# Attention's beginning in an attention, routed-experts and feed-forward kernel: the first head's operands written by engines, loads on two queues, hash operand in four operations, some thresholds behind the statistics

## The chip, the cores and the metric

The kernel runs on one core of one Trainium2 chip. The metric is the time of one execution on the device in microseconds (us), taken as the median of several runs. The chip has a tensor engine (PE), a vector engine (DVE), a scalar engine (ACT), GpSimd (POOL) and a sync engine (SP) whose queue only issues transfers here. Results of matrix products land in PSUM, everything else is kept in SBUF.

## The reference

Three stages follow one another; the change is in the first.

```python
def _attn_ref(q, k, v, proj):              # q, k, v: (2, 8, 768, 64), proj: (64, 6)
    q_bits = (einsum('bhsd,dk->bhsk', q, proj) > 0)
    k_bits = (einsum('bhsd,dk->bhsk', k, proj) > 0)
    mask = q_bucket[:, :, :, None] == k_bucket[:, :, None, :]     # bucket: the six bits as a number
    scores = where(mask, q @ k.T / sqrt(64), -1e9)
    attn = exp(scores - max); attn = attn / (sum(attn) + 1e-09)
    return attn @ v
...
x = attention output as (1536, 512)
x = moe(x)      # top 2 of 8 experts, 512 -> 1024 -> 512, gate with noise
return ffn(x)   # 512 -> 2048 -> 512, g = h * sigmoid(1.702 h)
```

## The kernel before

Attention walks over 16 heads, taken as 8 pairs. A head is worked in 6 steps of 128 query rows, 96 steps in all; n counts them. Each step does `scores(n)` (4 products into PSUM, L721), `statistics(n)` on DVE (a row maximum, L1080, and the small exp_arg, L1083), an exponential on ACT (L1386), `transposes(n)` on PE (6 of 128x128, L732), and their copy out by ACT (L1395). In the loop over n, PE issues scores(n + 2), then transposes(n), then a unit of the next pair if one is due, then every second step the product with V for the head before (L746). ACT runs one exponential ahead of the copies.

Scores are made from four stacks per head, QA, KA, QB and KB, each 128 rows by 768 columns inside the big weight tile W. QA and KA hold the high and low parts of Q and K (each fp32 number is split in two), so that two products give nearly full precision; QB and KB hold in their upper 64 rows the hash bits, as 0 or a large number, which push rows of different buckets apart.

A pair's operands are made in 8 units. Units 0 and 1 transpose the two halves of Q (L703), 2 and 3 those of K; ACT copies the high part out of PSUM (L1380) and DVE the rest, `lo = ps - hi` (L1064). Units 4 to 7 multiply the parts with the hash operand `hash_m` (L708), and DVE compares the result with a threshold, once for each head of the pair, and writes it into QB or KB (L1074). The high and low parts are then moved into the stacks by 12 transfers of 192 KB per pair on SP's queue (L461); a pair's first scores wait for all of them. Pair 0's units run before the loop; those of pair p + 1 run in steps 0 to 7 of pair p (`unit_at`).

SP's queue issues in program order: Q and K of pair 0 (L411), the projection twice (L446, L447), router weights and noise (L448 to L450), then for each pair the 12 moves, the next pair's Q and K, V (L416) and one chunk of expert weights into `staged` (L422). GpSimd scales Q in place, once per pair (L533), and behind the scaling of pairs 0 to 3 splits one staged chunk into high and low parts (`split_chunk`, L522 and L527). Pair p's units therefore wait on PE for GpSimd's scaling, and this stands in GpSimd's order behind the split of the chunk before.

Semaphores named below: `s_ud` counts units done by DVE, `s_unit` units issued by PE, `s_hi` high parts done by ACT, `s_stq` and `s_stk` the moves landed.

## Time and profile before

| | |
|---|---|
| median of 3 runs | 957.33 us (955.73 to 957.73) |
| the profiled execution | 957.01 us, its span 955.1 us |
| busy in the span | PE 892.1 us (93%), DVE 393.9, ACT 412.0, GpSimd 320.4 |
| attention | from the start to about 303 us |

The span is what the trace covers; about 2 us of the execution lie around it. A busy PE is the union of its pipelined products, not PE at its peak. Times in rows are microseconds from the span's start. "PEclk" is the granted clock of TensorE as a share of full speed.

### The profile page before, as it was taken

The page shows a single profiled execution, that of the slowest core. Times are in us where ns is not written, and L with a number is a line of the kernel's source. Part 1 is how long each engine was busy: PE and PEld are TensorE (multiplying, and loading weights), DVE is VectorE, ACT ScalarE, POOL GpSimd, SP SyncE. Part 2 cuts the span into 40 slices and gives each one's busy share as a digit, 9 for nine tenths or more (in the row PEclk, how much of TensorE's full clock was granted, in tenths as well). Part 3 has the DMA queues.
Part 4 walks back from the last instruction along what each step waited for, and adds up shares of the span by engine and source line. Part 5 has one row for each costly group of instructions (what it writes and reads, how often), then busy time and mean ns, then how long its engine had stood idle before and what let it go on. Part 6 is the DMA issues. An engine that isn't in the chain of part 4 may idle for free.

```text
span 955.1 us, 13447 instructions
## 1 busy us (share of the span) xinstructions
PE 892.1 (93%) x4966; PEld 778.9 (82%) x4966; DVE 393.9 (41%) x758; ACT 412.0 (43%) x695; POOL 320.4 (34%) x214
## 2 busy tenths in 40 slices
PE   2699999999999889999999999998899999999998
PEld 2566666676665689999999999998789998989986
DVE  4477676767774732122221222212233333333322
ACT  1576676676675323343443434421443323223222
POOL 1222020000060035676646566479564110100100
PEclk8699999999999979999999999999799999999999
DMA  7346525623432014666565544444343010000000
GB/s 157 98 124 171 122 79 142 169 69 84 116 111 86 26 41 142 200 200 222 173 198 190 179 160 155 138 155 130 119 157 89 33 44 22 33 0 0 34 1 33
DMA packets 69747, 105.13 MB, mean 110 GB/s; under 512 B 33364, under 2 KB 35412, under 8 KB 69684
## 3 DMA queue, kind: packets, MB, share of 16 engines
q1 hardware_dynamic: 56240, 74.32, 27.0%
q0 software_dynamic: 5488, 15.51, 5.1%
q10 hardware_dynamic: 7956, 14.49, 4.5%
q8 instruction: 36, 0.59, 0.2%
q14 instruction: 27, 0.22, 0.1%
HBM read 64.61 MB, written 20.81 MB: 89 GB/s over the span
## 4 chain that ended last, share of the span: by engine, by line
PE 84%; DVE 6%; issue 3%; ACT 2%; SPq 2%; DMA 1%; POOL 1%; ACTq 0%; DVEq 0%; POOLq 0%
PE psS L864 15%; PE psS L1003 14%; PE psS L1018 9%; PE psS L882 7%; PE psV L746 7%; PE psT L732 5%; PE psS L721 5%; PE psV L1018 5%; PE psV L882 4%; PE psM L882 4%; DVE W L1074 2%; PE psM L708 2%; PE psT L897 1%; ACT probT L1395 1%; PE psM L703 1%
## 5 line engine op out<-in xcount | busy, mean ns | idle before, releaser
L527 POOL TENSOR_TENSOR W<-staged,W 128x1024 fp32r<-128x1024 f32 x80 | 191.4, 2394 | 133.1 <-ACT W L1455 115.3
L864 PE MATMUL psS<-xT_hi,W 128*128 128x416 f32 x512 | 142.2, 359 | 1.1 <-DVE xT_lo L1270 1.1
L1003 PE MATMUL psS<-x2T_hi,W 128*128 (+1 forms) x512 | 134.5, 344 | 3.9 <-issue 3.9
L1386 ACT ACTIVATE prob<-psS,exp_arg 128x768 f32<-128x768 f32 x96 | 95.5, 994 | 37.1 <-DVE exp_arg L1083 37.0
L1080 DVE TENSOR_REDUCE neg_max<-psS 128x1 f32<-128x768 f32 x96 | 91.5, 953 | 45.9 <-PE psS L721 45.0
L721 PE MATMUL psS<-W 128*128 128x384 f32 x384 | 94.4, 369 | 11.7 <-DMA W<-k_hi 10.0
L1395 ACT ACTIVATE probT<-psT 128x768 f32<-128x768 f32 x96 | 78.0, 812 | 59.0 <-PE psT L732 57.4
L1003 PEld LDWEIGHTS psS<-x2T_hi,W 128*128 128x128 f32 x512 | 94.7, 191 | 9.4 <-issue 4.2
L1276 DVE SCALAR_TENSOR_TENSOR hT_lo<-psS,hT_hi 128x416 fp32r<-128x416 f32 x64 | 37.9, 592 | 155.9 <-ACT hT_hi L1448 155.9
L721 PEld LDWEIGHTS psS<-W 128*128 128x128 f32 x384 | 65.5, 196 | 38.9 <-issue 34.8
L864 PEld LDWEIGHTS psS<-xT_hi,W 128*128 128x128 f32 x512 | 92.8, 188 | 2.3 <-issue 1.2
L1344 DVE TENSOR_TENSOR g_sb<-psS,sig 128x384 f32<-128x384 f32 x64 | 35.7, 558 | 140.5 <-ACT sig L1529 140.5
L864 PE MATMUL psS<-xT_lo,W 128*128 128x416 f32 x256 | 90.2, 352 | 0.0
L1529 ACT ACTIVATE sig<-psS 128x384 f32<-128x384 f32 x64 | 31.4, 491 | 134.4 <-PE psS L1003 134.4
L1003 PE MATMUL psS<-x2T_lo,W 128*128 (+1 forms) x256 | 87.4, 341 | 0.0
L732 PE MATMUL psT<-ident,prob 128*128 128x128 f32 x576 | 80.7, 277 | 5.6 <-ACT probT L1395 5.6
L1455 ACT ACTIVATE W<-staged 128x1024 fp32r<-128x1024 f32 x67 | 70.7, 1055 | 34.0 <-issue 20.5
L732 PEld LDWEIGHTS psT<-ident,prob 128*128 128x128 f32 x576 | 67.4, 142 | 16.4 <-issue 13.2
L1018 PE MATMUL psS<-W,g_hi 128*128 128x512 f32 x256 | 79.9, 393 | 0.3 <-issue 0.3
L522 POOL TENSOR_TENSOR W<-staged,ones_col 128x1024 fp32r<-128x1024 f32 x13 | 24.6, 1894 | 137.4 <-DMA staged<-in_moe_w 97.4
L882 PE MATMUL psS<-hT_hi,W 128*128 128x416 f32 x256 | 69.5, 353 | 0.0
L746 PE MATMUL psV<-probT,v_raw 128*64 128x384 f32 x360 | 68.0, 499 | 0.0
(258 smaller groups left out, 1410.1 us busy)
## 6 DMA issues: line engine op xcount, KB each, us to landing
staged<-in_moe_w SPq DMA_DIRECT2D x64, 512.0 KB, 3.6
ys_dram<-x_sb ACTq DMA_DIRECT2D x68, 208.0 KB
W<-q_hi SPq DMA_DIRECT2D x32, 192.0 KB, 3.3
W<-k_hi SPq DMA_DIRECT2D x32, 192.0 KB, 3.7
staged<-in_moe_w_in SPq DMA_DIRECT2D x8, 512.0 KB, 3.4
staged<-in_moe_w_out SPq DMA_DIRECT2D x8, 512.0 KB, 3.6
q_raw<-in_q SPq DMA_DIRECT2D x16, 192.0 KB, 4.0
k_raw<-in_k SPq DMA_DIRECT2D x16, 192.0 KB, 3.7
```

The costliest lines, as they stand in the source:

```text
L527: nc.gpsimd.tensor_tensor(W[:, at + BLOCK:at + BLOCK + CH], staged[:, n % 2], W[:, at:at + CH].bitcast(F32), ALU.subtract).then_inc(s_spli ...
L721: last = nc.tensor.matmul(psS[:, n % 2, half, 0:HALF], stack(slot, a)[:, qt * P:(qt + 1) * P], stack(slot, b_)[:, half * HALF:(half + 1) * ...
L732: last = nc.tensor.transpose(psT[:, half, j * P:(j + 1) * P], prob[:, n % 2, c * P:(c + 1) * P], ident[:])
L746: last = nc.tensor.matmul(av_bank(hd)[half * D:(half + 1) * D, 0:HALF], v_raw[:, hd // 2 % 2, hd % 2, c * D:(c + 1) * D], probT[:, hd % 2, ...
L864: mm = nc.tensor.matmul(psS[:, 0, f % 2, 0:TM], W[:, at:at + P], x[:, t % 2, c], start=c == 0 and n == 0, stop=c == DC - 1 and n == 2)
L882: mm = nc.tensor.matmul(y_bank[d][:, 0:TM], W[:, at:at + P], h[:, f % 2], start=f == 0 and n == 0, stop=f == FC - 1 and n == 2)
L1003: mm = nc.tensor.matmul(psS[:, 0, f % 2, 0:GN], W[:, at:at + P], x[:, bass.ds(buf + c * GN, GN)], start=c == 0 and n == 0, stop=c == DC - ...
L1018: mm = nc.tensor.matmul(out_bank[j], gp[:, f % 2, j * P:(j + 1) * P], W[:, at:at + DM], start=f == 0 and n == 0, stop=f == GC - 1 and n == 2)
L1080: nc.vector.tensor_reduce(neg_max[:, o, 0:1], psS[:, o, :, 0:HALF], mybir.AxisListType.XY, ALU.max, negate=True).then_inc(s_stat, 1)
L1386: nc.scalar.activation(prob[:, o, :].rearrange("p (a c) -> p a c", a=2), psS[:, o, :, 0:HALF], ACT.Exp, bias=exp_arg[:, o, 0:1], scale=exp ...
L1395: nc.scalar.activation(probT[:, hd % 2, :, t * P:(t + 1) * P].rearrange("p (a c) q -> p a c q", a=2), psT[:, :, 0:HALF].rearrange("p a (c ...
L1455: A(W[:, at:at + CH], staged[:, n % 2], ACT.Copy).then_inc(s_whi if block < E else s_late, 1)
```

## The change

Only the beginning of attention is rewritten, and the scaling of Q for all pairs.

- Scaling: GpSimd's in-place scaling of q_raw is gone. ACT's copy of the Q units takes `scale=SCALE`, and DVE's low part of Q becomes `ps * SCALE - hi` in one operation. PE's unit 0 waits for the Q transfers themselves.
- First loads: SP issues head 0's Q, half of the projection and head 0's K; ACT's queue issues head 1's Q, the other half and head 1's K. Pair 1's Q and K come next on SP's queue; V, router weights, noise and the first staged chunk come behind pair 0's moves.
- Hash operand: four DVE operations of 64 x 24 (with a `sign` tile set ahead) in place of sixteen of 64 x 6.
- Pair 0's units use a PSUM bank each. Head 0's stacks are written by engines: GpSimd copies Q's high part into both halves of QA, ACT K's parts into KA and KB, DVE Q's low part into QB. Head 1's six parts still go by transfer, and `moved(pr)` counts them; `scores(6)`, head 1's first, waits for them.
- Thresholds: those of head 0 come first, in 4 operations; those of head 1 are put behind the statistics of steps 0 and 1.
- Pair 1's units are one step later in the loop (steps 1 to 8). PE also does 6 products that nobody reads (`unread`) at its start and 3 ahead of `scores(0)`.

```diff
 def unit_bank(u, first):
-    return psS[:, u // 2 % 2, u % 2] if first else psM
+    return (psS[:, 0, 0], psS[:, 0, 1], psS[:, 1, 0], psS[:, 1, 1], psT[:, 0], psT[:, 1], psV, psM)[u] if first else psM
+
+def moved(pr):
+
+    return max(96 * pr - 48, 0)
 def columns(t, buf, j):
...
 def unit_at(n):
-    return n // PS + 1, n % PS
+    return n // PS + 1, n % PS - (n < PS)
 def attention_over(eng):
...
-    load_qk(0)
+    sp.dma_start(q_raw[:, :, 0], q_v[0].rearrange("p (t d) -> p t d", d=D)).then_inc(s_q, 16)
     sp.dma_start(proj_sb[0:D, :], proj).then_inc(s_proj, 16)
-    sp.dma_start(proj_sb[D:P, :], proj).then_inc(s_proj, 16)
-    sp.dma_start(w_router[:, :, 0:E], w_gate.rearrange("(c p) e -> p c e", p=P)).then_inc(s_wr, 16)
-    sp.dma_start(w_router[:, :, E:2 * E], w_noise.rearrange("(c p) e -> p c e", p=P)).then_inc(s_wr, 16)
-    sp.dma_start(noise_sb[:].rearrange("p (b t) e -> p b (t e)", b=B),
-                 noise.rearrange("(b p t) e -> p b (t e)", b=B, t=NT)).then_inc(s_wr, 16)
+    sp.dma_start(k_raw[:, :, 0], k_v[0].rearrange("p (t d) -> p t d", d=D)).then_inc(s_k, 16)
+    load_qk(1)
     for pr in range(PAIRS):
         if pr >= 2:
             sp.wait_ge(s_S, PS * (pr - 1))
         for hi, lo, s, u in ((q_hi, q_lo, s_stq, 2), (k_hi, k_lo, s_stk, 4)):
             sp.wait_ge(s_ud, UNITS * pr + u)
-            for hh in range(2):
+            for hh in range(0 if pr else 1, 2):
                 rows, slot = slice(hh * D, (hh + 1) * D), 2 * (pr % 2) + hh
                 moves = (((QA, 0, hi), (QA, 1, hi), (QB, 0, lo)), ((KA, 0, hi), (KA, 1, lo), (KB, 0, hi)))[u // 2 - 1]
                 for which, at, src in moves:
                     sp.dma_start(stack(slot, which)[at * D:(at + 1) * D].bitcast(F32), src[rows].bitcast(F32)).then_inc(s, 16)
-        if pr + 1 < PAIRS:
+        if pr == 0:
+            load_v(0)
+            sp.dma_start(w_router[:, :, 0:E], w_gate.rearrange("(c p) e -> p c e", p=P)).then_inc(s_wr, 16)
+            sp.dma_start(w_router[:, :, E:2 * E], w_noise.rearrange("(c p) e -> p c e", p=P)).then_inc(s_wr, 16)
+            sp.dma_start(noise_sb[:].rearrange("p (b t) e -> p b (t e)", b=B),
+                         noise.rearrange("(b p t) e -> p b (t e)", b=B, t=NT)).then_inc(s_wr, 16)
+        elif pr + 1 < PAIRS:
             load_qk(pr + 1)
-        load_v(pr)
+        if pr:
+            load_v(pr)
         if pr < 6:
...
                                 ALU.subtract).then_inc(s_split, 1)
     pool.wait_ge(s_const, 16)
-    for pr in range(PAIRS):
-        pool.wait_ge(s_q, 32 * (pr + 1))
-        nc.gpsimd.tensor_scalar(q_raw[:], q_raw[:], SCALE, None, ALU.mult).then_inc(s_scaled, 1)
-        if pr < 4:
-            split_chunk(0, pr)
+    pool.wait_ge(s_hi, 2)
+    for which, at in ((QA, 0), (QA, 1)):
+        nc.gpsimd.tensor_scalar(stack(0, which)[at * D:(at + 1) * D], q_hi[0:D], 1.0, None, ALU.mult).then_inc(s_first, 1)
+    pool.wait_ge(s_first, 6)
+    for c in range(4):
+        split_chunk(0, c)
     pool.wait_ge(s_S, PS * (PAIRS - 1))
...
     def unit(pr, u, first=False):
         if u == 0:
-            pe.wait_ge(s_scaled, pr + 1)
+            pe.wait_ge(s_q, 32 * (pr + 1))
         if u == 2:
             pe.wait_ge(s_k, 32 * (pr + 1))
-        if u == 4 and first:
-            pe.wait_ge(s_hash, 18)
+        if u in (4, 6) and first:
+            pe.wait_ge(s_hash, u)
         if not first:
             pe.wait_ge(s_ud, UNITS * pr + u)
-        elif u >= 4:
-            pe.wait_ge(s_ud, u - 3)
+        elif u in (4, 6):
+            pe.wait_ge(s_ud, u - 2)
         side, half = (u // 2) % 2, u % 2
...
     def scores(n):
         slot, qt = (n // NT) % 4, n % NT
-        if n % PS == 0:
+        if n == 0:
+            pe.wait_ge(s_thr, 4)
+            pe.wait_ge(s_first, 6)
+        elif n == NT or n % PS == 0:
             pe.wait_ge(s_ud, UNITS * (n // PS + 1))
-            pe.wait_ge(s_stq, 96 * (n // PS + 1))
-            pe.wait_ge(s_stk, 96 * (n // PS + 1))
+            pe.wait_ge(s_stq, moved(n // PS + 1))
+            pe.wait_ge(s_stk, moved(n // PS + 1))
         at_least(pe, s_exp, n - 1)
...
     def transposes(n):
         pe.wait_ge(s_exp, n + 1)
         at_least(pe, s_evA, n)
+        if n == 0:
+            pe.wait_ge(s_ud, 6)
         for half in range(2):
...
             last = nc.tensor.transpose(av_bank(hd)[:, j * P:(j + 1) * P], oT(hd)[:, j * P:(j + 1) * P], ident[:])
         last.then_inc(s_back, 1)
+    def unread(n):
+
+        for i in range(n):
+            nc.tensor.matmul(psS[:, 0, 0, 0:P], ident[:], ident[:], start=True, stop=True)
+
     pe.wait_ge(s_const, 8)
+    unread(6)
     for u in range(UNITS):
         unit(0, u, True)
+    unread(3)
     for n in range(2):
...
             scores(n + 2)
         transposes(n)
         pr, u = unit_at(n)
-        if pr < PAIRS and u < UNITS:
+        if pr < PAIRS and 0 <= u < UNITS:
             unit(pr, u)
...
 @block.vector
 def _(dve):
+    for side in range(2):
+        for n in range(2):
+            nc.vector.memset(sign[:, side, n:n + 1], (1.0 / SCALE, 1.0)[side] * (1.0 if n == side else -1.0)).then_inc(s_sign, 1)
     dve.wait_ge(s_const, 16)
     dve.wait_ge(s_proj, 32)
-    nc.vector.tensor_copy(proj_hi[:], proj_sb[:]).then_inc(s_hash, 1)
+    nc.vector.tensor_copy(proj_parts[:, 0], proj_sb[:]).then_inc(s_hash, 1)
     dve.wait_ge(s_hash, 1)
-    nc.vector.tensor_tensor(proj_lo[:], proj_sb[:], proj_hi[:].bitcast(F32), ALU.subtract).then_inc(s_hash, 1)
+    nc.vector.tensor_tensor(proj_parts[:, 1], proj_sb[:], proj_parts[:, 0].bitcast(F32), ALU.subtract).then_inc(s_hash, 1)
     dve.wait_ge(s_hash, 2)
-    hi, lo = proj_hi[:].bitcast(F32), proj_lo[:].bitcast(F32)
-    for hh in range(2):
-        rows = slice(hh * D, (hh + 1) * D)
-        for m, src in enumerate((hi, lo)):
-            bit, opposite = (slice(hh * D + n * bits, hh * D + (n + 1) * bits) for n in range(2))
-
-            for side, cols in enumerate(((bit, opposite), (opposite, bit))):
-                size = (1.0 / SCALE, 1.0)[side]
-                nc.vector.tensor_scalar(hash_m[rows, side, m, cols[0]], src[rows], size, None, ALU.mult).then_inc(s_hash, 1)
-                nc.vector.tensor_scalar(hash_m[rows, side, m, cols[1]], src[rows], -size, None, ALU.mult).then_inc(s_hash, 1)
-
-    def unit(pr, u, first=False):
+    dve.wait_ge(s_sign, 4)
+    for side in range(2):
+        for hh in range(2):
+            rows = slice(hh * D, (hh + 1) * D)
+            nc.vector.tensor_tensor(hash_m[rows, side, :, hh * D:hh * D + 2 * bits].rearrange("p m (n b) -> p m n b", n=2),
+                                    proj_parts[rows, :, None, :].bitcast(F32).to_broadcast([D, 2, 2, bits]),
+                                    sign[rows, side, None, :, None].to_broadcast([D, 2, 2, bits]), ALU.mult).then_inc(s_hash, 1)
+
+    def unit(pr, u, first=False, heads=(0, 1)):
         ps = unit_bank(u, first)
         if u < 4:
             c = slice((u % 2) * HALF, (u % 2 + 1) * HALF)
             dve.wait_ge(s_hi, 4 * pr + u + 1)
             hi, lo = ((q_hi, q_lo), (k_hi, k_lo))[u // 2]
-            last = nc.vector.tensor_tensor(lo[:, c], ps[:, 0:HALF], hi[:, c].bitcast(F32), ALU.subtract)
+            if u < 2:
+                last = nc.vector.scalar_tensor_tensor(lo[:, c], ps[:, 0:HALF], SCALE, hi[:, c].bitcast(F32), ALU.mult, ALU.subtract)
+            else:
+                last = nc.vector.tensor_tensor(lo[:, c], ps[:, 0:HALF], hi[:, c].bitcast(F32), ALU.subtract)
         else:
...
             if u == 4:
                 at_least(dve, s_S, PS * (pr - 1))
             t, s, w = ((thrQ, sclQ, QB), (thrK, sclK, KB))[side]
-            for hh in range(2):
+            for hh in heads:
                 rows = slice(hh * D, (hh + 1) * D)
                 last = nc.vector.tensor_scalar(stack(2 * (pr % 2) + hh, w)[D:P, c], ps[rows, 0:HALF], t[rows], s[rows], ALU.is_gt, ALU.mult)
-        last.then_inc(s_ud, 1)
+        last.then_inc(s_ud if 1 in heads else s_thr, 1)
     def statistics(n):
...
                                 row_rec[:, hd % 2].rearrange("p (a j) -> p a j", a=2)[:, :, :, None].to_broadcast([P, 2, NT // 2, D]),
                                 ALU.mult).then_inc(s_norm, 1)
-    for u in range(UNITS):
+    for u in range(4):
         unit(0, u, True)
+        if u == 1:
+            dve.wait_ge(s_ud, 2)
+            nc.vector.tensor_copy(stack(0, QB)[0:D], q_lo[0:D].bitcast(F32)).then_inc(s_first, 1)
+    for u in range(4, UNITS):
+        unit(0, u, True, (0,))
     for n in range(2):
         statistics(n)
+        for u in (2 * n + 4, 2 * n + 5):
+            unit(0, u, True, (1,))
     for n in range(STEPS):
...
             normalise(hd - 2)
         if n:
             pr, u = unit_at(n - 1)
-            if pr < PAIRS and u < UNITS:
+            if pr < PAIRS and 0 <= u < UNITS:
                 unit(pr, u)
...
         c = slice((u % 2) * HALF, (u % 2 + 1) * HALF)
         act.wait_ge(s_unit, UNITS * pr + u + 1)
         if u in (0, 2) and not first:
-            act.wait_ge((s_stq, s_stk)[u // 2], 96 * pr)
-        nc.scalar.activation((q_hi, k_hi)[u // 2][:, c], unit_bank(u, first)[:, 0:HALF], ACT.Copy).then_inc(s_hi, 1)
+            act.wait_ge((s_stq, s_stk)[u // 2], moved(pr))
+            act.wait_ge(s_first, 6)
+        nc.scalar.activation((q_hi, k_hi)[u // 2][:, c], unit_bank(u, first)[:, 0:HALF], ACT.Copy,
+                             scale=SCALE if u < 2 else 1.0).then_inc(s_hi, 1)
     def exponentials(n):
...
         nc.scalar.activation(probT[:, hd % 2, :, t * P:(t + 1) * P].rearrange("p (a c) q -> p a c q", a=2),
                              psT[:, :, 0:HALF].rearrange("p a (c q) -> p a c q", q=P), ACT.Copy).then_inc(s_evA, 1)
+    act.dma_start(q_raw[:, :, 1], q_v[1].rearrange("p (t d) -> p t d", d=D)).then_inc(s_q, 16)
+    act.dma_start(proj_sb[D:P, :], proj).then_inc(s_proj, 16)
+    act.dma_start(k_raw[:, :, 1], k_v[1].rearrange("p (t d) -> p t d", d=D)).then_inc(s_k, 16)
     for u in range(4):
         unit(0, u, True)
+    act.wait_ge(s_hi, 4)
+    for which, at, src, done in ((KA, 0, k_hi, 0), (KB, 0, k_hi, 0), (KA, 1, k_lo, 4)):
+        at_least(act, s_ud, done)
+        nc.scalar.activation(stack(0, which)[at * D:(at + 1) * D], src[0:D].bitcast(F32), ACT.Copy).then_inc(s_first, 1)
     exponentials(0)
     for n in range(STEPS):
         if n + 1 < STEPS:
             exponentials(n + 1)
         evac(n)
         pr, u = unit_at(n)
-        if pr < PAIRS and u < 4:
+        if pr < PAIRS and 0 <= u < 4:
             unit(pr, u)
```

On DVE at the start of the program, before the change: the hash operand, the low parts, eight threshold operations, then the statistics.

```order
3 L1055 TENSOR_SCALAR hash_m<-proj_hi 64x6 [waits s_hash]
...
19 L1064 TENSOR_TENSOR q_lo<-psS,q_hi 128x384 [waits s_hi] x2
20 L1064 TENSOR_TENSOR k_lo<-psS,k_hi 128x384 [waits s_hi] x2
21 L1074 TENSOR_SCALAR W<-psS,thr 64x384 [waits s_unit]
22 L1074 TENSOR_SCALAR W<-psS,thr 64x384
...
28 L1074 TENSOR_SCALAR W<-psS,thr 64x384
29 L1080 TENSOR_REDUCE neg_max<-psS 128x1 [waits s_S]
30 L1083 SCALAR_TENSOR_TENSOR exp_arg<-neg_max 128x2 [waits s_stat]
```

The same place with the change (line numbers are those of the changed file).

```order
4 L1079 TENSOR_TENSOR hash_m<-proj_parts,sign 64x2x12 [waits s_sign,s_hash]
5 L1079 TENSOR_TENSOR hash_m<-proj_parts,sign 64x2x12 x3
6 L1090 SCALAR_TENSOR_TENSOR q_lo<-psS,q_hi 128x384 [waits s_hi] x2
7 L1136 CAST W<-q_lo 64x768 [waits s_ud]
8 L1092 TENSOR_TENSOR k_lo<-psS,k_hi 128x384 [waits s_hi] x2
9 L1102 TENSOR_SCALAR W<-psT,thr 64x384 [waits s_unit] x2
10 L1102 TENSOR_SCALAR W<-psV,thr 64x384 [waits s_unit]
11 L1102 TENSOR_SCALAR W<-psM,thr 64x384 [waits s_unit]
12 L1108 TENSOR_REDUCE neg_max<-psS 128x1 [waits s_S]
13 L1111 SCALAR_TENSOR_TENSOR exp_arg<-neg_max 128x2 [waits s_stat]
14 L1102 TENSOR_SCALAR W<-psT,thr 64x384 [waits s_unit] x2
15 L1108 TENSOR_REDUCE neg_max<-psS 128x1 [waits s_S]
```

Four threshold operations have moved behind statistics, a copy of 64 x 768 stands between the low parts of Q and of K, and twelve small operations are gone.

On GpSimd behind its constants, before:

```order
20 L533 TENSOR_SCALAR q_raw<-q_raw 128x768 [waits s_q,s_const]
21 L522 TENSOR_TENSOR W<-staged,ones_col 128x1024 [waits s_stage0]
22 L527 TENSOR_TENSOR W<-staged,W 128x1024 [waits s_whi]
23 L533 TENSOR_SCALAR q_raw<-q_raw 128x768 [waits s_q]
24 L522 TENSOR_TENSOR W<-staged,ones_col 128x1024 [waits s_stage1]
```

and with the change:

```order
20 L545 TENSOR_SCALAR W<-q_hi 64x768 [waits s_hi,s_const]
21 L545 TENSOR_SCALAR W<-q_hi 64x768
22 L534 TENSOR_TENSOR W<-staged,ones_col 128x1024 [waits s_stage0,s_first]
23 L539 TENSOR_TENSOR W<-staged,W 128x1024 [waits s_whi]
24 L534 TENSOR_TENSOR W<-staged,ones_col 128x1024 [waits s_stage1]
```

The scalings have gone from between the splits; the two copies into QA stand ahead of the first split.

On PE ahead of the loop, before:

```order
1 L703 MATMUL psS<-ident,q_raw 128x128 [waits s_scaled,s_const]
...
17 L721 MATMUL psS<-W 128x384 [waits s_stk,s_stq,s_ud]
18 L721 MATMUL psS<-W 128x384 x7
19 L721 MATMUL psS<-W 128x384 [waits s_exp]
20 L721 MATMUL psS<-W 128x384 x3
21 L732 MATMUL psT<-ident,prob 128x128 [waits s_exp]
22 L732 MATMUL psT<-ident,prob 128x128 x5
23 L703 MATMUL psM<-ident,q_raw 128x128 [waits s_ud,s_scaled]
```

and with the change:

```order
1 L779 MATMUL psS<-ident 128x128 [waits s_const]
2 L779 MATMUL psS<-ident 128x128 x5
3 L716 MATMUL psS<-ident,q_raw 128x128 [waits s_q]
...
18 L779 MATMUL psS<-ident 128x128 x3
19 L737 MATMUL psS<-W 128x384 [waits s_first,s_thr]
...
23 L750 MATMUL psT<-ident,prob 128x128 [waits s_ud,s_exp]
24 L750 MATMUL psT<-ident,prob 128x128 x5
25 L737 MATMUL psS<-W 128x384 [waits s_exp]
26 L737 MATMUL psS<-W 128x384 x3
```

`scores(0)` waits for the engines' copies and head 0's thresholds and no longer for transfers, and pair 1's first unit has gone from behind `transposes(0)`.

## Rows read from the trace of the kernel before

**Rows 1.** The page's head.

```profile
span 955.1 us, 13447 instructions
```

**Rows 2.** Timeline from 0: start, length, engine, line, operation, output and inputs, count.

```profile
0.81 1.38 SPq L411 DMA_DIRECT2D q_raw<-in_q  x2
...
3.62 1.01 SPq L446 DMA_DIRECT2D proj_sb<-in_proj  x1
...
5.34 2.16 POOL L533 TENSOR_SCALAR q_raw<-q_raw 128x768 f32<-128x768 f32 x1 [1.60 <-DMA q_raw<-in_q]
...
6.99 0.54 DVE L1043 CAST proj_hi<-proj_sb 128x6 fp32r<-128x6 f32 x1 [6.99 <-DMA proj_sb<-in_proj]
...
7.64 1.51 PE L703 MATMUL psS<-ident,q_raw 128*128 128x128 f32 x6 [7.64 <-POOL q_raw L533]
...
8.55 1.13 ACT L1380 ACTIVATE q_hi<-psS 128x384 fp32r<-128x384 f32 x2 [6.45 <-PE psS L703]
...
9.19 1.08 DVE L1064 TENSOR_TENSOR q_lo<-psS,q_hi 128x384 fp32r<-128x384 f32 x2
```

**Rows 3.** Timeline from 11 to 26.

```profile
11.59 5.59 DVE L1074 TENSOR_SCALAR W<-psS,thr 64x384 fp32r<-64x384 f32 x8
...
18.49 0.77 SPq L461 DMA_DIRECT2D W<-k_hi  x1
...
22.73 2.90 PE L721 MATMUL psS<-W 128*128 128x384 f32 x8 [10.03 <-DMA W<-k_hi]
...
24.39 0.96 DVE L1080 TENSOR_REDUCE neg_max<-psS 128x1 f32<-128x768 f32 x1 [7.21 <-PE psS L721]
```

**Rows 4.** Stretches: their length, engines' busy us (instructions), granted clock, DMA share, GB/s.

```profile
16.00:18.00 2.00, 0.00 (x0) 0.00 (x0) 1.16 (x2) 0.00 (x0) 0.00 (x0) 0.88 0.98 238
...
38.00:40.00 2.00, 2.00 (x12) 1.91 (x10) 1.38 (x3) 0.90 (x3) 0.00 (x0) 0.50 0.00 0
...
40.80:42.00 1.20, 1.20 (x9) 1.11 (x8) 0.94 (x2) 1.11 (x3) 0.00 (x0) 0.75 0.00 0
```

**Rows 5.** Timeline from 29 to 37.

```profile
29.78 1.89 POOL L522 TENSOR_TENSOR W<-staged,ones_col 128x1024 fp32r<-128x1024 f32 x1 [22.29 <-DMA staged<-in_moe_w]
...
36.24 0.90 PE L703 MATMUL psM<-ident,q_raw 128*128 128x128 f32 x3 [6.60 <-POOL q_raw L533]
```

**Rows 6.** Groups by line and shape, whole span: count, then busy us, mean ns, idle before.

```profile
L1386 ACT ACTIVATE prob<-psS,exp_arg 128x768 f32<-128x768 f32 x96 | 95.5, 994 | 37.1 <-DVE exp_arg L1083 37.0
...
L1455 ACT ACTIVATE W<-staged 128x1024 fp32r<-128x1024 f32 x67 | 70.7, 1055 | 34.0 <-issue 20.5 <-DVE x_sb L1291 6.5 <-DMA staged<-in_moe_w 6.2
...
L1276 DVE SCALAR_TENSOR_TENSOR hT_lo<-psS,hT_hi 128x416 fp32r<-128x416 f32 x64 | 37.9, 592 | 155.9 <-ACT hT_hi L1448 155.9
...
L1270 DVE TENSOR_TENSOR xT_lo<-psT,xT_hi 128x416 fp32r<-128x416 f32 x28 | 16.6, 592 | 60.1 <-ACT xT_hi L1442 60.1
```

**Rows 7.** Timeline, DVE and POOL, around 62 and around 268.

```profile
62.21 2.37 POOL L527 TENSOR_TENSOR W<-staged,W 128x1024 fp32r<-128x1024 f32 x1
62.82 1.77 DVE L1083 SCALAR_TENSOR_TENSOR exp_arg<-neg_max 128x2 f32<-128x2 f32 x1
...
268.31 1.54 DVE L1083 SCALAR_TENSOR_TENSOR exp_arg<-neg_max 128x2 f32<-128x2 f32 x1
269.80 1.89 POOL L522 TENSOR_TENSOR W<-staged,ones_col 128x1024 fp32r<-128x1024 f32 x1
```

**Rows 8.** Timeline, PE: the transposes of steps 2, 6, 7, 8 and 9.

```profile
41.42 0.82 PE L732 MATMUL psT<-ident,prob 128*128 128x128 f32 x6
...
49.97 0.82 PE L732 MATMUL psT<-ident,prob 128*128 128x128 f32 x6
...
52.55 0.82 PE L732 MATMUL psT<-ident,prob 128*128 128x128 f32 x6
...
56.77 0.82 PE L732 MATMUL psT<-ident,prob 128*128 128x128 f32 x6
...
58.58 0.85 PE L732 MATMUL psT<-ident,prob 128*128 128x128 f32 x6 [0.30 <-ACT probT L1395]
```

14 lines of the change are left out of this document (9 added, 5 removed).

## The prediction

> **What bounds the kernel now.** I read the page's head, then the timeline of the beginning, then the clock by stretches. The span is 955.1 us and the profiled execution 957.01 [rows 1], so 1.9 us lie around it. PE is busy nearly everywhere but in the first 42 us, and there the reader is to see three losses. First, scores(0) start at 22.73, and PE had stood idle 10.03 us for the last stack transfer [rows 3]. Second, PE stands again at 36.24, after 6.60 us of waiting for the scaled Q of pair 1: GpSimd does that scaling behind the split of chunk 0, whose first operation starts at 29.78 when the transfer has landed [rows 5]. Third, in the first idle time the granted clock falls (0.88 over 16 to 18, so from full to half, 2.4 to 1.2 GHz) and is at half until about 41.4 [rows 4]. From step 2 on, steps run at 2 to 2.6 us, or about 2.4 with V's product, and all that follows attention hangs on its end; I found nothing later that is tied to a time of its own. So the change is worth what it moves the transposes of step 9, which stand at 58.58 [rows 8] and are the first ahead of which all of pair 1's units are done in either kernel.
>
> **Stage A, to scores(0).** Q: before, the two transfers were issued by 2.19 and GpSimd was released by the second at 5.34 [rows 2], 3.15 after. Issued at once on two queues at 0.81 they should be there at 1.5 + 3.15 = 4.7. (A stack transfer of the same size, issued by 19.26, released PE at 22.73, 3.5 after [rows 3]; that would give 5.0.) The 2.16 of scaling is gone, so PE starts at 4.7 and not at 7.64. From PE's start to the first q_hi is 0.91 (7.64 to 8.55) and both halves take 1.13 [rows 2]: q_hi is there at 6.8. DVE's low parts come 0.6 behind, done at 7.4. The projection is second in its queue, about 2 us earlier than the 3.62 of before [rows 2], so near 4.9; its six small operations are done ahead of 6.2. K is third in each queue, issued by about 3.1, there near 6.5; k_hi is done at about 8.8. The scaling by ACT's copy is an immediate and I cost it at nothing; DVE's three-operand form takes 592 ns at 416 columns, just as the two-operand one [rows 6], so nothing in the seven later pairs either.
>
> GpSimd begins its two copies of 768 columns at 6.8. The nearest row is the scaling, same columns on twice the partitions, 2.16 [rows 2]: the first ends at 9.0. DVE asks for its copy into QB at 7.4. Here the trace speaks: the CAST of six columns, issued while GpSimd was scaling, took 0.54 and ended at 7.53, when GpSimd ended (7.50) [rows 2], and the exp_arg of two columns took 1.77 and ended at 64.59 with GpSimd's 62.21 + 2.37 [rows 7]. So DVE's SBUF-to-SBUF copy waits to 9.0. In a run of GpSimd operations it gets in between two: one ended at 269.85 as GpSimd's next began at 269.80 [rows 7]. Its own time lies between nothing much (the small CAST, once free) and the 0.96 that DVE takes to read 768 columns [rows 3]; I take 0.9, the row with its column count. So 9.9. The low parts of K stand behind it, 1.1 (as 1.08 for Q's, [rows 2]): 11.0. Then four thresholds at 5.59 / 8 = 0.70 each [rows 3]: 2.8, so 13.8. Units 6 and 7 on PE need K's low parts but are done in time for the third threshold. ACT's copies into KA and KB: 1055 ns for 1024 columns [rows 6], so about 0.85; the last, of k_lo, ends near 12. GpSimd's second copy, pushed by DVE's, ends near 12.1. All lie under the thresholds. **scores(0) at 13.8 and not 22.73: 8.9 gained.** Without GpSimd in the way the copy is done by 8.3, k_lo waits for k_hi to 9.4, and scores(0) come at 12.2. If the copy waits for both of GpSimd's, k_lo is done at 13.1 and scores(0) come at 15.9.
>
> The Trainium skill (SBUF — State Buffer, section "SBUF: two separate sides") says that DVE in a two-port mode and GpSimd hold the shared ports by an exclusive lock for a whole instruction; the two rows agree. It speaks against putting these two copies side by side. The skill (VectorE: DVE Perf Modes, "Mode 2×_2P — use both read ports for one tensor") also has an fp32 SBUF-to-SBUF copy at two elements a cycle, by which QB's copy is an estimated 0.45 and the sum 0.45 shorter; no row of before has such a copy at length.
>
> **The clock.** Before, PE had done nothing since 12.7 (22.73 less 10.03 [rows 3]) when the clock fell between 16 and 18 [rows 4]. With the change PE runs unread products from about 2.3, units from 4.7 to 9.3, again from 11.0 to about 12.6, and scores from 13.8, with pauses of under 2 us, so I take the full clock from scores(0) on.
>
> **Stage B, scores(0) to the transposes of step 2.** Before, 41.42 − 22.73 = 18.7 [rows 3, 8], 6.60 of it the wait, most of the rest at half clock. After, counted from scores(0): four products 1.0 (half the 2.90 for eight at half clock [rows 3], less the clock's share), the maximum 0.96, exp_arg 0.2, so exp(0) ends at 3.2; DVE meanwhile does two of head 1's thresholds (1.4) to 3.6, the second statistics to 4.8; exp(1) (0.99 [rows 6]) to 5.8; scores(3) to 6.8; DVE's other two thresholds to 6.2 and statistics(2) to 7.3; exp(2) behind the copy out of step 0, to about 8.4; scores(4), and the transposes of step 2 at 9.3. That is 23.1 on the clock. **9.4 gained.** Were the four moved thresholds free it would be 8; at half clock some 12.
>
> **Stage C, steps 2 to 9.** Before 58.58 − 41.42 = 17.16 [rows 8]. The change makes it longer: seven units fall in it where six did, and the last (hash products and two thresholds) now falls in a step that had none. A threshold step takes 52.55 − 49.97 = 2.58, a bare one 58.58 − 56.77 = 1.81 [rows 8]: 0.8 lost, less than that if the freed q/k step gives some back; 0.6. Chunk 0's split (1.89 and 2.37 [rows 5, 7]) lay in PE's second idle time. That cover is gone: before, it landed 10.5 behind the end of the last move's issue (19.26 to 29.78 [rows 3, 5]); the last move is now issued by 14.6 and fewer transfers follow it, so GpSimd splits at some 23 to 27.5, in steps 2 to 4. Each of its operations can hold an exp_arg as the 1.77 above. Two holds cost at most 3.5, and nothing if ACT is not yet ready for the exponential; ACT still has a copy out to do there, so I take 0.5, near the low end. **1.1 lost.**
>
> Of what moves on queues: pair 1's Q and K are issued by about 10, long ahead of their units at 21 and later. Head 1's six moves stand behind them, issued from 9.9 to 14.6 at 0.77 each [rows 3], landed by 19; PE asks at scores(6), near 26.5. V and staged only get earlier. GpSimd's lost scalings release nobody else.
>
> **Sum.** 8.9 + 9.4 − 1.1 = 17.2. Against the profiled execution 957.01 − 17.2 = 939.8. The median of the runs shown is 957.33, 0.3 above, inside their spread; I name 939.8.
>
> **Rivals.**
> - QB's copy waits for both of GpSimd's copies: scores(0) at 15.9, 2.1 later, **941.9**. For it: back to back operations with nothing to wait for between them; against it: the row at 268.31. Chance 0.13.
> - No hold at all, or the copy at 0.45 with everything ahead a little earlier: scores(0) at 12.2, **938.2**. Against it: both rows of holds. 0.12.
> - The clock is at half in the first steps after all, because PE works in short bursts with waits between: stage B 12, so **942.5**. For it: before, it stayed at half through steps 0 and 1, and still over 38 to 40, where PE was busy 2.00 of 2.00 us [rows 4]. 0.08.
> - Chunk 0's split costs both holds in full: **942.8**. 0.06.
> - The gain is given back behind attention, at a transfer or at the clock in the idle parts of routing: half of it, **948**. Nothing in the rows speaks for it. 0.03.
> - Slower than before: head 1's moves. If they land late, PE stops at scores(6). They would have to land later than 26.5 + 17.2 = 43.7, that is 29 us after their issue; at 50 the time is **963**. The same transfers took 3.5 [rows 3]. 0.01.
> - That the change does not do what it says would be scores(0) still waiting for a transfer; its waits name only the engines' copies and thresholds, and I give it 0.01, at **950**.
>
> **Chances and range.** The forecast, 938.8 to 941, has 0.56. The two nearest rivals and those of 942.5 and 942.8 lie within 936.5 to 944, which holds about 0.85; errors of stage C and of the landing of Q, up to 1 us each, are in it. What a measurement can tell from no change is 0.2%, 1.9 us. Every case but two lies below 955.4: faster 0.98, same 0.01, slower 0.01.
>
> **What would show it.** In the trace after: PE's first transposes at 4.7 (landing of Q), a CAST into QB of about 2.5 us that ends with GpSimd's first copy, the low parts of K behind it, scores(0) near 13.8 behind the fourth threshold, a granted clock of 1.00 throughout, no wait for pair 1's Q, two exp_args of more than 1 us between 23 and 28, the transposes of step 9 near 41.4, and all later stages as long as before. The forecast is wrong if Q lands later on two queues than on one, if the clock drops, or if a later stage is not moved rigidly.

## The result, and the profile after

The changed kernel takes 934.32 us (median of 4 runs, 933.12 to 934.78) beside 957.53 for the kernel before (955.73 to 958.29): ratio 0.9762, interval 0.975 to 0.9774. That is 23.2 us less where 17.2 were predicted, and below the range of 936.5 to 944. The profiled execution of 934.65 us has a span of 932.9, which is 22.2 under that of [rows 1]; below it is followed mark by mark.

First the timeline of the changed kernel up to scores(0), to be held against [rows 2, 3] (start, length, engine, line, operation, output and inputs):

```profile
4.83 0.17 DVE L1071 CAST proj_parts<-proj_sb 128x6 fp32r<-128x6 f32 x1 [3.78 <-DMA proj_sb<-in_proj]
...
5.08 1.49 PE L716 MATMUL psS<-ident,q_raw 128*128 128x128 f32 x6
...
5.97 1.13 ACT L1416 ACTIVATE q_hi<-psS 128x384 fp32r<-128x384 f32 x2 [1.53 <-PE psS L716]
...
6.49 1.20 DVE L1090 SCALAR_TENSOR_TENSOR q_lo<-psS,q_hi 128x384 fp32r<-128x384 f32 x2 [0.45 <-ACT q_hi L1416]
...
7.28 4.36 POOL L545 TENSOR_SCALAR W<-q_hi 64x768 fp32r<-64x768 f32 x2 [3.54 <-ACT q_hi L1416]
...
7.72 0.81 DVE L1136 CAST W<-q_lo 64x768 fp32r<-64x768 f32 x1
...
8.46 1.00 DVE L1092 TENSOR_TENSOR k_lo<-psS,k_hi 128x384 fp32r<-128x384 f32 x2
...
9.49 1.25 DVE L1102 TENSOR_SCALAR W<-psT,thr 64x384 fp32r<-64x384 f32 x2
...
11.26 0.66 DVE L1102 TENSOR_SCALAR W<-psM,thr 64x384 fp32r<-64x384 f32 x1
...
11.97 1.66 PE L737 MATMUL psS<-W 128*128 128x384 f32 x8 [0.41 <-DVE W L1102]
...
16.11 0.82 PE L750 MATMUL psT<-ident,prob 128*128 128x128 f32 x6
```

DVE is busy without a gap from the low parts of Q (6.49) to the last threshold (11.92), and that sets scores(0) at 11.97, not 22.73. QB's cast began while GpSimd's first copy (7.28 to about 9.46) ran, and ended well inside it. Eight products of scores take 1.66, not the 2.90 of [rows 3]: the granted clock is full. The marks of [rows 8], for steps 2, 7 and 9, and the two operations of chunk 0's split against [rows 5], with the two exp_args that they held (timeline, PE, POOL and DVE):

```profile
21.13 0.82 PE L750 MATMUL psT<-ident,prob 128*128 128x128 f32 x6
...
21.82 1.89 POOL L534 TENSOR_TENSOR W<-staged,ones_col 128x1024 fp32r<-128x1024 f32 x1 [10.17 <-DMA staged<-in_moe_w]
...
22.83 0.89 DVE L1111 SCALAR_TENSOR_TENSOR exp_arg<-neg_max 128x2 f32<-128x2 f32 x1
...
23.79 2.37 POOL L539 TENSOR_TENSOR W<-staged,W 128x1024 fp32r<-128x1024 f32 x1
...
25.09 1.08 DVE L1111 SCALAR_TENSOR_TENSOR exp_arg<-neg_max 128x2 f32<-128x2 f32 x1
...
32.82 0.82 PE L750 MATMUL psT<-ident,prob 128*128 128x128 f32 x6
...
38.94 0.82 PE L750 MATMUL psT<-ident,prob 128*128 128x128 f32 x6
```

Stretches of the changed kernel, as in [rows 4]: the clock column is 1.00 where before it was 0.88, 0.50 and 0.75.

```profile
16.00:18.00 2.00, 1.12 (x9) 0.85 (x8) 1.90 (x5) 1.33 (x3) 0.00 (x0) 1.00 0.95 237
38.00:40.00 2.00, 2.00 (x15) 1.67 (x15) 1.88 (x6) 1.89 (x4) 0.00 (x0) 1.00 0.94 233
40.80:42.00 1.20, 1.20 (x9) 0.83 (x6) 0.46 (x2) 0.67 (x1) 0.00 (x0) 1.00 0.81 323
```

From scores(0) to step 2's transposes 9.16 (18.69 before), from there to step 9's 17.81 (17.16). So 10.76 + 9.53 − 0.65 = 19.6 are gained by step 9, and the experts start 19.8 earlier. The other 2.4 come at one place I had not looked at, between the experts and the feed-forward stage. Timeline of before there, then of the changed kernel:

```profile
668.40 0.63 PE L1032 MATMUL psM<-ident,yg 128*128 128x128 f32 x4 [2.66 <-issue]
...
671.45 0.60 ACT L1523 ACTIVATE x2T_hi<-psM 128x512 fp32r<-128x512 f32 x1 [4.79 <-issue]
```

```profile
648.53 0.63 PE L1057 MATMUL psM<-ident,yg 128*128 128x128 f32 x4 [2.67 <-issue]
...
649.19 0.60 ACT L1567 ACTIVATE x2T_hi<-psM 128x512 fp32r<-128x512 f32 x1 [2.42 <-PE psM L1057]
```

PE's product begins 19.87 earlier, ACT's copy of it 22.26 earlier. Before, ACT stood 3.05 behind the product's start and its idle time is put down to "issue", to nothing the profile shows; after, 0.66, and the product released it.

### The profile page after: what moved, and what is told of

Read it like the earlier page. It is cut to its first block, busy times and chain, and to the rows that moved or that the text cites. A ratio compares the mean times of both kernels' runs of the same rounds, so it can differ in the third digit from the quotient of the medians.

```text
span 932.9 us, 13476 instructions
## 1 busy us (share of the span) xinstructions
PE 891.1 (96%) x4984; PEld 776.9 (83%) x4984; DVE 394.2 (42%) x751; ACT 414.6 (44%) x698; POOL 307.7 (33%) x208
## 4 chain that ended last, share of the span: by engine, by line
PE 85%; DVE 8%; issue 3%; ACT 3%; POOL 1%; DMA 0%; ACTq 0%; POOLq 0%; DVEq 0%
PE psS L889 15%; PE psS L1028 15%; PE psS L1043 10%; PE psS L907 7%; PE psV L764 7%; PE psS L737 5%; PE psV L1043 5%; PE psT L750 5%; PE psV L907 4%; PE psM L907 4%; DVE W L1102 3%; PE psM L721 2%; PE psT L922 1%; DVE neg_max L1108 1%; ACT probT L1432 1%
## 5 line engine op out<-in xcount | busy, mean ns | idle before, releaser
L737 PE MATMUL psS<-W 128*128 128x384 f32 x384 | 91.2, 360 | 4.4 <-ACT prob L1423 3.6
L737 PEld LDWEIGHTS psS<-W 128*128 128x128 f32 x384 | 62.9, 189 | 32.4 <-issue 25.5
```

What stands on the lines that cost most here:

```text
L737: last = nc.tensor.matmul(psS[:, n % 2, half, 0:HALF], stack(slot, a)[:, qt * P:(qt + 1) * P], stack(slot, b_)[:, half * HALF:(half + 1) * ...
```

## The experiments

Times are medians, "mark 9" is the start of step 9's transposes in the profiled execution (58.58 before, 38.94 with the change), and ratios are to the kernel before, measured beside it. Executions of one kernel differ: those of the changed kernel by up to 2.3 us, those of others by up to 4.8 (a_dmabusy2), and marks by some tenths. A profiled execution can be the slowest or the fastest of its kernel; where it is, the text says so. The changed kernel run once more gave this.

> The changed kernel itself, unaltered, beside the other one: 934.3, span about 932.5, QB's cast again 0.81 and x2T_hi again 0.66 behind PE's product.

933.73 (932.37 to 934.70, ratio 0.9757, interval 0.9743 to 0.977), mark 9 at 38.34. Differences under 1 us between kernels below are not read.

Part of this spread lies in one place, behind ACT's first copy into x2T_hi, with which the feed-forward stage begins. The stretches of 6 us there, for the changed kernel and for the same kernel run again:

```profile
650.00:656.00 6.00, 4.42 (x15) 4.21 (x14) 1.72 (x3) 1.82 (x3) 4.32 (x3) 0.50 0.51 169
```

```profile
650.00:656.00 6.00, 3.76 (x24) 3.55 (x23) 2.23 (x4) 2.67 (x5) 5.24 (x4) 1.00 0.53 166
```

At half clock it is 33.2 us from that copy to the first one of the next group, at full clock 31.8. Over all traces it is 31.4 to 31.8 where the clock stayed full in the 6 us behind the copy, 33.2 to 33.7 where it was mostly at half, and 32.2 to 32.5 where it was at 0.83 to 0.86.

### The 2.4 us between experts and feed-forward

ACT reaches x2T_hi over code that it skips (the branches for expert tiles beyond those used). Counted in ACT's program, that instruction is number 1605 before and 1629 with the change. I moved it by waits that are already met, and changed nothing else.

```diff
+            for _ in range(24):
+                act.wait_ge(s_const, 1)
```

These stand ahead of ACT's first copy, in the kernel before.

> The kernel before with 24 waits that are already met, put on ACT's queue while it idles ahead of its first copy, so that everything behind stands at the same place in ACT's program as in the changed kernel. Theory (the 2.4 us that came behind the experts is a stop of ACT's sequencer that depends on where the code behind the skipped branches lies in its program): ACT's first copy into x2T_hi starts 0.7 us after PE's product and not 3.0, time 2.3 us under before, about 955.0. Rival (the stop depends on the moment or on the transfers in flight, which the earlier start has moved): unchanged, 957.3, the copy still starts 3 us after the product.

954.80 (median of 10, 0.9978, 0.9968 to 0.9987): 2.1 us gained by 24 waits that do nothing. As expected, x2T_hi stands 0.67 behind its product:

```profile
669.13 0.63 PE L1032 MATMUL psM<-ident,yg 128*128 128x128 f32 x4 [2.33 <-issue]
...
669.80 0.60 ACT L1525 ACTIVATE x2T_hi<-psM 128x512 fp32r<-128x512 f32 x1 [2.08 <-PE psM L1032]
```

The reverse, on the changed kernel: 13 waits fewer inside attention, and 232 more behind `preload_act_table(ACT.Sigmoid)`.

> The changed kernel with 13 waits fewer on ACT (the wait for the engines' copies stands only at pair 1's first Q unit). The code behind the experts' skipped branches then lies 11 instructions behind its place in before, 13 ahead of its place in the changed kernel. Theory of the place in the program: either as the changed kernel, 934.3, or with the stop back, 936.6, nothing between. Rival (moment or transfers in flight): 934.3, as nothing ahead of it is moved.

935.05 (0.9781), x2T_hi (now number 1616) 0.66 behind: no stop.

> The changed kernel with 232 waits that are already met put on ACT between routing and the experts, where ACT stood idle for 23 us. Nothing of attention moves; ACT's first x2T_hi, instruction 1629 of its program in the changed kernel, becomes 1861, which is 256 behind the 1605 that it was in the kernel before. Theory (the 2.4 us are a stop of ACT's sequencer that depends on where the code behind the skipped branches lies in ACT's program, and the place counts in blocks that divide 256): x2T_hi starts some 3 us behind PE's product and not 0.66, idle 'issue', and the time is 936.5 to 937. Rival (the stop has another cause, in attention's new beginning): x2T_hi still 0.66 behind the product and 934.3.

938.65 (0.98, 0.9784 to 0.9816), above the expectation. The stop is back, 3.29 behind the product:

```profile
651.71 0.63 PE L1057 MATMUL psM<-ident,yg 128*128 128x128 f32 x4 [2.45 <-issue]
...
655.00 0.60 ACT L1569 ACTIVATE x2T_hi<-psM 128x512 fp32r<-128x512 f32 x1 [4.83 <-issue]
```

It accounts for 2.6 of the 4.3 us that this kernel loses; in its profiled execution (940.42, above its median) 3.2 more are lost ahead of 651, of which 0.75 by mark 9. That rest I did not settle. The three traces with a stop of 3 us or more (before, b_scale, a_late232) all have the clock at half behind it and the 33.2 to 33.3 us named above; among the seventeen others, the short and the long times both occur. So a stop may cost a further 1.4 to 1.9 us through the clock; three traces do not prove it.

Over all runs whose rows I read: numbers 1605 (before, and the kernel with only the scaling changed) and 1861 have 3.05 to 3.56, numbers 1616 to 1629 have 0.66 to 0.67, but for 1626 (first loads on one queue) with 1.19. So the place in ACT's program decides whether the stop comes, and attention's beginning does not. What ACT does in the stop stays open: a fetch of its instructions is a guess from "issue" behind skipped code, and no row shows it.

### What GpSimd holds

The prediction had QB's cast held to the end of GpSimd's first copy. First GpSimd's copies were given a second input:

```diff
-nc.gpsimd.tensor_scalar(stack(0, which)[...], q_hi[0:D], 1.0, None, ALU.mult)
+nc.gpsimd.tensor_tensor(stack(0, which)[...], q_hi[0:D].bitcast(F32), ones_col[0:D].to_broadcast([D, S]), ALU.mult)
```

> The changed kernel with GpSimd's two copies into QA done as a product of q_hi with a column of ones, two inputs in place of one; everything else as it was. Theory (only GpSimd operations with two inputs hold DVE's SBUF-to-SBUF work, which is why the QB copy ran free inside a one-input copy): the CAST into QB takes about 2 us, to the end of GpSimd's first copy near 9.5, scores(0) near 13.3, time 935.3 to 936. Rival (no GpSimd operation holds this CAST, since it runs at one element a cycle): CAST 0.81, scores(0) near 12.0 (a little later if GpSimd's two-input form is slower), 934.3.

934.99 (0.9761), scores(0) at 12.24, both less than expected for two inputs. The cast took 1.33 (7.47 to 8.80), longer than 0.81, but the copies had become shorter (3.20 for the two, begun at 6.92, in place of 4.36), so little was lost. For a clean reading I put a measuring part ahead of the changed kernel.

> The changed kernel with a measuring part ahead of it: 20 pairs of one GpSimd and one DVE operation, DVE's begun some 0.5 us after GpSimd's. GpSimd: nothing, the in-place scaling of 128x768, the copy of 64x768 into a stack, a product with a column of ones (128x768, as the split's first operation), a subtraction (as its second). DVE in each: the cast of 64x768 to fp32r (QB's), the cast of 128x6, the exp_arg operation, a copy of 64x768 that stays fp32. Theory (only GpSimd operations with two tensor inputs hold DVE): durations equal beside nothing, scaling and copy, 0.8 or less for the casts and 0.1 to 0.2 for the small ones, and well over 1 us beside the product and the subtraction. Rival 1 (the prediction's: any GpSimd operation holds any SBUF-to-SBUF operation of DVE): over 1 us in all four. Rival 2 (the cast is never held, only other forms are): the casts constant in all five. The time itself is some 40 to 60 us above the changed kernel's, for the measuring part.

It missed its aim: nearly every DVE operation began just ahead of GpSimd's. It gave the durations alone (0.55 for the cast of 64x768, 0.17 and 0.16 for the small ones), and that GpSimd's 2.12 became 2.49 beside such a cast. With DVE's operation asked for later:

> The measuring part again, with DVE's operation put behind 50 (first 20 pairs) and 110 (last 20) tiny writes into PSUM, so that it is asked for inside GpSimd's operation; in the first measurement nearly every one began just ahead of it. What that one showed: alone, the cast and the copy of 64x768 take 0.55 and not 0.8, and a GpSimd operation beside them takes 0.37 longer (2.49 for 2.12). Theory (a shared port, held by DVE's fast cast for its whole length, but given back by one-input GpSimd operations at some point inside them): beside the scaling and the copy the casts take 0.55 to 1.3, beside the product and the subtraction the exp_arg operation ends with them. Rival 1 (the prediction's, whole GpSimd operations hold everything): each DVE operation ends with GpSimd's. Rival 2 (GpSimd holds only the small operations with two inputs): casts 0.55 throughout.

Timeline of that part, three of its pairs, without DVE's tiny writes: a copy of 64x768 inside a scaling, and the cast and an exp_arg inside a subtraction.

```profile
20.25 2.13 POOL L537 TENSOR_SCALAR prob<-prob 128x768 f32<-128x768 f32 x1 [0.22 <-DVE psM L1097]
21.03 0.55 DVE L1108 COPY prob<-W 64x768 f32<-64x768 f32 x1
...
40.58 1.80 POOL L543 TENSOR_TENSOR W<-prob,W 128x768 fp32r<-128x768 f32 x1 [0.95 <-DVE psM L1097]
41.81 0.98 DVE L1101 CAST W<-W 64x768 fp32r<-64x768 f32 x1
...
45.18 1.80 POOL L543 TENSOR_TENSOR W<-prob,W 128x768 fp32r<-128x768 f32 x1 [0.31 <-DVE psM L1097]
46.77 0.23 DVE L1105 SCALAR_TENSOR_TENSOR probT<-probT 128x2 f32<-128x2 f32 x1
```

All six DVE operations asked for inside two-input GpSimd operations ended just behind them (the big ones 0.41, the small ones 0.01 to 0.03 behind), all eight inside one-input operations were not held. The six had been asked for 0.79 to 1.59 in, the eight 0.78 to 1.22 in. The last 20 pairs did not overlap.

> 24 pairs of one GpSimd operation with one tensor input (12 times the in-place scaling of 128x768, 12 times the copy of 64x768 into a stack) and one DVE operation asked for at six distances behind its start, from about 0.2 to 1.7 us: the cast of 64x768 (0.55 alone) and the cast of 128x6 (0.17 alone). Theory (such a GpSimd operation of 2.12 us keeps DVE's SBUF-to-SBUF work out in its first 0.84 us and again from about 1.44 to its end, and lets it in between; read from the QB cast, 0.44 in, which took 0.81; one 0.04 in, 1.21; four at 0.78 to 0.95 in, not held; the six-column cast of the kernel before, 1.65 in, held to the end): casts asked for at 0.2 and 0.5 end 0.41 behind 0.84, those at 0.8 to 1.2 take 0.55, and those at 1.5 and 1.7 end 0.41 behind GpSimd's end; the small casts likewise with 0.03 in place of 0.41. Rival (one-input GpSimd operations never hold; the longer durations came from something else): 0.55 and 0.17 in all 24.

Its timeline, again without the tiny writes, one-input scalings with a cast asked for 0.26, 0.09, 0.87, 1.21 and 1.56 in:

```profile
4.73 2.16 POOL L534 TENSOR_SCALAR prob<-prob 128x768 f32<-128x768 f32 x1 [0.97 <-DVE psM L1090]
4.99 1.00 DVE L1094 CAST W<-W 64x768 fp32r<-64x768 f32 x1
...
7.11 2.13 POOL L534 TENSOR_SCALAR prob<-prob 128x768 f32<-128x768 f32 x1 [0.22 <-DVE psM L1090]
7.20 0.75 DVE L1096 CAST W<-prob 128x6 fp32r<-128x6 f32 x1
...
16.49 2.13 POOL L534 TENSOR_SCALAR prob<-prob 128x768 f32<-128x768 f32 x1 [0.22 <-DVE psM L1090]
17.36 0.17 DVE L1096 CAST W<-prob 128x6 fp32r<-128x6 f32 x1
...
18.84 2.44 POOL L534 TENSOR_SCALAR prob<-prob 128x768 f32<-128x768 f32 x1 [0.22 <-DVE psM L1090]
20.05 0.55 DVE L1094 CAST W<-W 64x768 fp32r<-64x768 f32 x1
...
21.50 2.13 POOL L534 TENSOR_SCALAR prob<-prob 128x768 f32<-128x768 f32 x1 [0.22 <-DVE psM L1090]
...
23.06 0.59 DVE L1096 CAST W<-prob 128x6 fp32r<-128x6 f32 x1
```

Ends behind GpSimd's start: 1.26, 0.84, then free, free (and GpSimd's own end pushed by 0.31), and 2.15, held to the end. The copies of 64x768 gave the same to 0.03, and with a cast asked for 1.75 in, an end 0.41 behind theirs. So a one-input GpSimd operation of this length (2.12 us) holds DVE's SBUF-to-SBUF work in its first 0.84 us, lets it in when asked for 0.72 to 1.22 in, and holds it again from a point between 1.22 and 1.56 on. An estimate of that point is 1.45: the cast begun 1.21 in ended 1.76 in and pushed GpSimd's end by 0.31. That explains the case's own rows: QB's cast asked for 0.44 in ended at 8.53, which is 0.84 + 0.41 behind 7.28; the six-column cast of [rows 2], 1.65 in, was held to the end.

### What the parts of the change are worth

Only the scaling, in the kernel before (ACT's `scale=SCALE` for Q, DVE's three-operand low part, no GpSimd scaling, PE waits for Q itself):

> The kernel before with only the scaling changed: GpSimd's scaling gone, ACT copies with a factor, DVE's low part of Q in the three-operand form; PE's unit 0 waits for the transfers. Theory: the 6.60 us wait at unit 0 of pair 1 goes, scores(0) hardly move because the stack moves on SP's queue follow the hash operations and the low parts, so about 6.6 to 9 us gained (the second idle time also kept the clock at half): 948.5 to 950.5. Rival: pair 1's Q itself lands late and takes the place of the wait, 2 to 4 gained: 953.5 to 955.5.

950.05 (0.9935, 0.9918 to 0.9951), 6.8 gained and within expectation. Its profiled execution was the fastest of four (947.35), with mark 9 at 48.11. The wait of PE for pair 1's Q is gone, and x2T_hi, at its old number 1605, still stops (3.56). Timeline of PE, and the stretches:

```profile
22.01 2.90 PE L719 MATMUL psS<-W 128*128 128x384 f32 x8 [10.35 <-DMA W<-k_hi]
...
30.67 0.84 PE L730 MATMUL psT<-ident,prob 128*128 128x128 f32 x6
```

```profile
24.00:26.00 2.00, 0.92 (x4) 0.41 (x3) 1.81 (x4) 1.08 (x2) 0.00 (x0) 0.75 0.96 312
26.00:28.00 2.00, 2.00 (x15) 1.97 (x16) 1.07 (x3) 1.43 (x3) 0.00 (x0) 1.00 0.42 171
```

From scores(0) to step 2's transposes it is 8.66, less than the 9.16 of the whole change: the clock is at half at first, but full again from 26 on, and all thresholds lie ahead of scores(0).

The unread products left out (`unread(6)`, `unread(3)`):

> The changed kernel without the nine unread products groups (six at PE's start, three ahead of scores(0)). Theory (the full clock in the first steps does not rest on them, PE's units and scores suffice once the 10 us stand is gone): within 0.5 us, 934 to 935, clock 1.00 throughout. Rival (they hold the clock): half clock in steps 0 to 2, 1.5 to 4 us slower, 936 to 938.5.

935.07 (0.9772), scores(0) at 12.15, clock full. The difference of 0.75 us is not read, so no gain by them is shown.

All eight thresholds ahead of scores(0):

> The changed kernel with head 1's four thresholds put back ahead of scores(0). Theory (DVE is the path to scores(0), and behind it the same four operations stand on the path of the first two steps): scores(0) 4 x 0.62 = 2.5 later, at 14.5, the stage to the transposes of step 2 shorter by what DVE no longer does there, 1.3 to 2.5 of 9.2, so the time 934.3 to 935.5. Rival (the moved thresholds are free behind the statistics): stage unchanged, time 936.8.

937.96 (0.9803, 0.9786 to 0.9819): 3.6 lost, above both. scores(0) came at 14.55, as expected, but PE had then stood idle for 2.97 and the clock was at half:

```profile
14.55 2.90 PE L738 MATMUL psS<-W 128*128 128x384 f32 x8 [2.97 <-DVE W L1103]
```

The next stage took 10.46, not 9.16 or less: what DVE no longer did there was lost again to the clock. b_scale is the comparison for this: there too all eight thresholds lie ahead of scores(0), but the clock was full again 4 us behind scores(0) and here only 9.5 us behind (0.50 until 24), and the stage was 8.66. At mark 9 this kernel is 3.0 behind the changed one.

All six first loads on SP's queue:

> The changed kernel with all six first loads on SP's queue, in the order Q, Q, projection, projection, K, K. ACT's program is 3 instructions shorter (x2T_hi at 1626, no stop expected). The second Q is issued at 1.5 in place of 0.83, the second K at 4.3 in place of 2.5. Theory (Q and K are on the path): PE's first transposes 5.1 to 5.7, K near 7.5 to 8, scores(0) 0.6 to 1.3 later, time 935 to 935.6. Rival (landing is bound elsewhere): scores(0) near 12.0, 934.3.

935.87 (0.9791, 0.9775 to 0.9807), a little above expectation. Q came as early (5.09), K 1.25 later, at 7.71, and scores(0) at 12.36, since QB's cast lies in that time. At step 9 it was 0.1 behind; the profiled execution (935.11) lost 0.5 more at x2T_hi, which stands 1.19 behind its product where no stop was expected.

Head 0's stacks by six more transfers, no engine copies:

```diff
-                    for hh in range(0 if pr else 1, 2):
+                    for hh in range(2):
...
-                    pe.wait_ge(s_first, 6)
+                    pe.wait_ge(s_stq, 96)
+                    pe.wait_ge(s_stk, 96)
```

> The changed kernel with head 0's stacks written by six more transfers, as before the change, and no copies by engines; loads, scaling, hash operand, thresholds and unread products stay. ACT's program is kept at the same length (1628 for 1629). SP issues the moves from about 9.3 on at 0.65 to 0.77 each, so the last lands near 21 and scores(0) start near 21, 9 us later than 11.97. Theory (the engine copies are worth the delay and the clock both): PE idle for 10 us, the granted clock at half through steps 0 and 1, stage to the transposes of step 2 about 12 and not 9.2, time 934.3 + 9 + 3 = 946 to 947. Rival (the clock in the changed kernel does not depend on this idle time): 943.5.

944.96 (943.48 to 947.80, ratio 0.9864), between theory and rival. In the profiled execution, the slowest of four, scores(0) came at 22.34 and mark 9 at 51.72. So of the parts taken out the engine copies are the largest, 10.6 us. The clock was at half through the stage behind scores(0), which took 12.66.

> The kernel with head 0's stacks by transfer, and 67 products that nobody reads ahead of scores(0) in place of 3, so that PE is busy until about 20. Theory (what that kernel loses beyond the later scores(0) is the clock): full clock from scores(0) on, the stage to the transposes of step 2 again near 9.2, time 943 to 944, that is 3 us less than with 3 such products. Rival: no difference between the two.

947.16 (0.9898). I had sized the filler wrongly: 67 of these products took 15.1 us, and scores(0) came at 24.90. Refitted:

> Head 0's stacks by transfer, with 50 products that nobody reads ahead of scores(0). With 67 they took 15.1 us and pushed scores(0) from 22.3 to 24.9; 50 should end near 21.3, ahead of the last move. Theory (the clock is worth about 2 us in the first steps): scores(0) near 22.3, full clock there, 10.6 us to the transposes of step 2 in place of 12.7, transposes of step 9 near 49.8 in place of 51.7, time 943. Rival (no difference from 3 such products): 945.

945.35 (0.9879), scores(0) at 23.36. No gain. In the profiled execution, 3.9 above the median, one exp_arg was held for 2.35 by chunk 0's split, PE stood idle behind it, and the clock fell in the same steps that the filler was to protect. So I moved the split away (`pool.wait_ge(s_S, 8)` ahead of it) in both:

> Head 0's stacks by transfer, 3 unread products, and GpSimd's split of chunk 0 not begun before scores(7), so that it holds no exp_arg in the first steps. Against the same with the split where it was (944.96): the clock still at half from scores(0), stage to the transposes of step 2 about 12.1 (12.66 less its share of holds), time about 944.5 to 946.

> The same with 50 unread products, so that only the clock at scores(0) differs from the kernel beside it. Theory (the clock is worth 2 to 3 us in the first steps once no hold breaks them up): full clock throughout, stage about 9.2 to 9.6, time 2 to 3 us below the kernel with 3 such products. Rival (the first steps are bound by DVE and ACT, and the clock is worth under 1 us): difference under 1 us.

944.99 and 944.47 (0.9887 and 0.9875; the intervals overlap). With 3 products the stage took 10.07, at half clock until 30, with 50 it took 9.46; but the clock fell there too (0.66 over 24 to 26, 0.50 behind), and the last transfer had landed 1.5 us later. The filler therefore never gave the clean comparison. What can be said is that at half clock and without a hold the stage is 10.07, against 9.16 at full clock with the change, and with all thresholds ahead of scores(0) 10.46 (a_thr8) against 8.66 (b_scale, full from 26 on). So in these profiled executions half clock costs this stage about 0.9 to 1.8 us.

Last, the changed kernel with the same move of the split:

> The changed kernel with GpSimd's split of chunk 0 not begun before scores(7). In the changed kernel it held two exp_args (0.89 and 1.08 in place of 0.16, in steps 2 to 4). Theory (these holds cost what the prediction took, about 0.5 us in steps 2 to 9): 933.5 to 934.2 where the changed kernel has 934.3, the two holds moved to a later step. Rival (ACT is not yet ready there, or the holds cost the same later): no difference to the changed kernel beside it.

933.49 (0.9757, 0.9744 to 0.977) beside 933.73: no difference. Step 5's transposes came at 27.26 and not 27.57, but by step 7 both stood at 32.3: the split now began at 27.56 and held the exp_arg at 28.97 (0.50). No kernel was run without any hold.

These parts do not add up to the whole: the scaling was put into the kernel before, the others taken out of the changed one. The hash operand in four operations and the PSUM banks were not taken out alone, so what they are worth is not known.

## Why the prediction was wrong, step by step

**Stage A** was to gain 8.9 and gained 10.76. Q landed later than said (5.08 for 4.7) and its low parts ended at 7.69 for 7.4. The step that failed is "DVE's SBUF-to-SBUF copy waits to 9.0", with "I take 0.9" for its own time: 2.5 in the sum, 0.84 measured (from the end of Q's low parts to the end of the cast). The rows were read rightly as holds, but carried over to a case they do not show. The exp_arg of [rows 7] stood beside a two-input operation, which held DVE to its end in each of the six pairs measured; the cast of [rows 2] fell into the second hold of a one-input one. And the cast's own time alone is 0.55. Here the Trainium skill (VectorE: DVE Perf Modes, "Mode 2×_2P — use both read ports for one tensor") was nearer than the row I chose: the estimate worked out from its two elements a cycle was 0.45 against 0.55 measured, while I took 0.9 from the reduction's 0.96. Its lock "for the whole instruction" (SBUF — State Buffer, "SBUF: two separate sides") agrees with the two-input operations and not with the one-input ones, which were open from 0.84 to at least 1.22. The lesser terms: thresholds 2.43 for 2.8, the low parts of K 0.93 for 1.1. Of 5.59 / 8 in [rows 3], part was particular to before, where heads alternated between the partition halves; now four in a row start in the same one (a_thr8's second four took 2.49, and no kernel changed this order alone, so that reason is argued only). The rival "no hold, or the copy at 0.45", scores(0) at 12.2, was closest, though there was a hold.

**The clock** was right: full from scores(0) on. The unread products, named first among its reasons, are not needed: without them it stays full as well, with PE idle for 1.08 ahead of scores(0). Idle for 2.97 there (a_thr8) the clock was at half. Between the two the rows do not agree: behind 2.10 (a_dmabusy2) scores(0) ran at full clock, behind 1.91 (a_dmabusy8) the clock fell over 24 to 26. So what keeps it is not shown beyond this.

**Stage B**: 9.4 predicted, 9.53 gained. The steps came as summed, exp(0) ended 3.19 behind scores(0) for 3.2. The scaling alone is worth all of it: b_scale shortened this stage by 10.03, the wait of 6.60 for pair 1's Q and the half clock behind that wait. The whole change, with the moved thresholds in this stage, gives 0.5 of it back (9.16 for 8.66), for what they save in stage A. The rival "half clock, 12" was sized too dear: 10.07 in a_dma8. The 12.66 of a_dma had a hold of the split in it.

**Stage C**: 1.1 to be lost, 0.65 lost. That two exp_args would be held is right (0.89 and 1.08), at 22.8 and 25.1. Their cost is about 0.3 of it: in a_split8 step 5 came that much earlier, and its own hold lost it again at step 7.

**"All that follows attention hangs on its end"**, and nothing later would change its length: this step failed, and it is nearly half of the miss (2.39 of 5.2 us in the profiled executions): ACT's stop at x2T_hi, which the sum had at nothing. I had looked for things tied to a time of their own, and found none. This stop is tied to the place of an instruction in ACT's program, which every added or removed instruction ahead of it moves. The row was there before (4.79 of idle time, "issue") and I had not asked what it was. That the change moved it to a place without the stop is luck; no part of the change aims at it.

**The sum**: 957.01 − 10.76 − 9.53 + 0.65 − 2.39 = 934.98, which leaves 0.3 of the profiled 934.65 to small changes on the way. Head 1's moves did not delay scores(6), pair 1's Q was not waited for, and neither the gain given back nor the loss came about.

## What to carry to other kernels

When a span ends in a chain with "issue" on it, ask for each such piece what stands there; one behind skipped code can come or go with any edit, by more than the edit is worth, so compare that gap first when a time surprises. Cost a copy beside GpSimd by how many inputs GpSimd's operation has and how far in the copy is asked for, and measure DVE's copy by itself before costing it by a reduction. And a filler must be sized from its own duration: what it delays is lost in full.

## What the runs showed of the hardware that I had not expected

- A one-input GpSimd operation of 768 columns (2.12 us) holds DVE's SBUF-to-SBUF work only in its first 0.84 us and from about 1.45 (an estimate, between 1.22 and 1.56) to its end (m_hold2, m_hold3). A DVE copy of 0.55 begun 1.14 to 1.22 in lengthened it by 0.25 to 0.32, one begun 0.79 in did not.
- 24 waits already met on ACT made the kernel before 2.1 us faster, with ACT's first instruction behind skipped branches then 0.67 behind its product's start and not 3.05.
- With PE kept busy by 50 unread products, the last of the same 12 transfers landed at 23.4 and 23.6 and not at 22.1 and 22.3 (4.9 to 5.0 us behind the end of its issue in place of 3.7 to 4.3). These are two executions each, and I did not find out why.
- The feed-forward stage begins at full or at half clock from one execution of the same kernel to the next, worth 1.4 us there (profiled executions of 934.65 and 933.73).
